# Second output product as three 256-column matmuls per group into one 256-column sum

## What is computed

```python
sig = 1.0 / (1.0 + np.exp(-f_logit))
f = lower_bound + (1.0 - lower_bound) * sig
h = f[:, t] * h + (1 - f[:, t]) * x[:, t]        # for every token t; y[:, t] = h
h1 = y @ w_in;   y1  = np.maximum(0.01 * h1, h1) @ w_out           # 256 -> 2048 -> 256
h2 = y1 @ w_in2                                                     # 256 -> 2048
g2 = np.where(h2 >= 1, h2, np.where(h2 <= -1, 0, (h2 + 1) ** 2 / 4))
out = g2 @ w_out2                                                   # 2048 -> 256
```

## Time and profile before

| | |
|---|---|
| median of 3 runs | 1105.47 us (1104.82 to 1106.61) |
| profiled execution, first to last instruction (span) | 1101.2 us |
| TensorE matmuls busy | 1078.7 us, 98%, 6156 matmuls, as many weight loads |
| VectorE busy | 813.1 us, 74% |
| ScalarE busy | 577.0 us, 52% |
| L686, 512 columns | 768 matmuls, 392 ns mean record |
| L691, 256 columns | 768 matmuls, 280 ns mean record |

### The profile page before, as it was taken

The page is one execution under the profiler, slowest core; times in us unless marked ns, Lnnn a source line. Parts: engine busy times, 40 slices in busy tenths (PEclk is TensorE's granted clock), DMA queues, the critical chain, the costliest instruction groups (busy, mean ns, idle before and its releaser), DMA issues.

```text
span 1101.2 us, 18595 instructions
## 1 busy us (share of the span) xinstructions
PE 1078.7 (98%) x6156; PEld 1041.4 (95%) x6156; DVE 813.1 (74%) x1542; ACT 577.0 (52%) x1210; POOL 42.7 (4%) x40
## 2 busy tenths in 40 slices
PE   4899999999999999999999999999999999999998
PEld 3899999999999999999999999999999999999997
DVE  5877777777777777777777777777777777777675
ACT  4545555555555555555555555555555555555453
POOL 5540000000000000000000000000000000000000
PEclk9999999999999999999999999999999999999999
DMA  5611020010100101010010200102001010000000
GB/s 166 172 54 30 1 44 1 14 29 14 29 0 16 27 14 29 0 29 14 14 29 0 43 0 14 29 0 43 0 14 29 14 24 0 14 0 15 1 15 13
DMA packets 105878, 27.36 MB, mean 25 GB/s; under 512 B 94272, under 2 KB 104704, under 8 KB 105856
## 3 DMA queue, kind: packets, MB, share of 16 engines
q1 hardware_dynamic: 104416, 22.36, 9.6%
q0 software_dynamic: 1440, 4.72, 1.3%
HBM read 20.84 MB, written 6.23 MB: 25 GB/s over the span
## 4 chain that ended last, share of the span: by engine, by line
PE 94%; DVE 3%; DMA 1%; SPq 1%; ACT 1%; issue 1%; DVEq 0%; ACTq 0%
PE H L657 47%; PE S L670 23%; PE S L686 16%; PE S L691 8%; SPq L254 1%; DMA bound<-in_lower_bound_dram 1%; DVE W L463 1%; DVE xT L495 0%; DMA raw<-in_moe_w_out_dram 0%; ACT W L331 0%; DVE X L510 0%; DVE H L536 0%; ACT G L389 0%; DVE G L542 0%; DVE late L528 0%
## 5 line engine op out<-in xcount | busy, mean ns | idle before, releaser
L657 PE MATMUL H<-X,W 128*128 (+2 forms) x1536 | 313.1, 339 | 13.9 <-DVE G L542 5.8
L657 PE MATMUL H<-Y,W 128*128 (+2 forms) x1536 | 309.3, 336 | 0.1
L670 PE MATMUL S<-G,W 128*128 128x384 f32 (+1 forms) x1536 | 308.3, 336 | 0.7 <-DVE Y L519 0.7
L382 ACT ACTIVATE leak<-H 128x384 f32<-128x384 f32 (+1 forms) x256 | 125.0, 488 | 321.8 <-PE H L657 311.5
L657 PEld LDWEIGHTS H<-X,W 128*128 128x128 f32 x1536 | 259.5, 189 | 27.2 <-issue 6.1
L686 PE MATMUL S<-W,G 128*128 128x512 f32 x768 | 278.1, 392 | 0.0
L670 PEld LDWEIGHTS S<-G,W 128*128 128x128 f32 x1536 | 270.8, 188 | 1.1 <-DVE G L542 1.0
L657 PEld LDWEIGHTS H<-Y,W 128*128 128x128 f32 x1536 | 270.2, 188 | 1.3 <-DVE G L564 0.8
L550 DVE SCALAR_TENSOR_TENSOR quad<-quad 128x384 f32<-128x384 f32 (+1 forms) x248 | 139.9, 564 | 118.3 <-ACT quad L396 118.2
L536 DVE TENSOR_TENSOR H<-H,leak 128x384 f32<-128x384 f32 (+1 forms) x256 | 143.6, 561 | 111.9 <-ACT leak L382 110.2
L691 PE MATMUL S<-W,G 128*128 128x256 f32 x768 | 214.9, 280 | 0.0
(11 more groups left out here) (38 smaller groups left out, 235.1 us busy)
## 6 DMA issues: line engine op xcount, KB each, us to landing
out_dram<-late SPq DMA_DIRECT2D x15, 384.0 KB, 2.4
stage_f<-in_f_logit_dram SPq DMA_DIRECT2D x56, 96.0 KB, 2.8
stage_x<-in_x_dram SPq DMA_DIRECT2D x56, 96.0 KB, 2.9
late<-in_moe_w_in_dram POOLq DMA_DIRECT2D x8, 256.0 KB, 3.2
late<-in_moe_w_out_dram POOLq DMA_DIRECT2D x8, 256.0 KB, 4.4
raw<-in_moe_w_in_dram SPq DMA_DIRECT2D x7, 256.0 KB, 4.2
raw<-in_moe_w_out_dram SPq DMA_DIRECT2D x7, 256.0 KB, 4.2
stage_f<-in_f_logit_dram SPq DMA_DIRECT2D x1, 384.0 KB, 3.4
```

The lines of the kernel that those rows point to most:

```text
L382: nc.scalar.activation(leak[:, 0:n], h1_bank(i, c)[:, 0:n], ACT.Copy, scale=0.01).then_inc(s_leak, 1)
L657: last = nc.tensor.matmul(bank[:, 0:n], w_in(W, a, c, k), V[:, parity(tile), b, k, 0:n], start=(k == 0 and (a, b) == PARTS[0]), stop=(k == ...
L670: last = nc.tensor.matmul(S1[:, d, 0:n], w_out(W1, a, c)[:, d * P:(d + 1) * P], G1[:, c % RING, b, 0:n], start=(c == 0 and (a, b) == PARTS ...
```

## The change

The two matmuls per group become the three of `PARTS`, each of 256 columns, all into `S2[:, g, 0:256]`: high G2 x high weights, high G2 x low weights, low G2 x high weights. The high part of G2 is now loaded twice per group. The columns 256 to 511 of the banks are no longer used, ScalarE's `cross_terms` with its buffer and semaphore is gone, and VectorE copies the sum to `result` in place of adding, waiting for TensorE's semaphores itself.

```diff
-        cross, result = late[:, 0], late[:, 1]
+        result = late[:, 1]
...
-            def cross_terms(tile):
-
-                reached(act, s_result, GROUPS * tile)
-                for g in range(GROUPS):
-
-                    if g < GROUPS - 1:
-                        act.wait_ge(s_sum2, (GROUPS - 1) * tile + g + 1)
-                    else:
-                        act.wait_ge(s_g2_used, CHUNKS * tile + CHUNKS)
-                    nc.scalar.activation(cross[:, g, :], S2[:, g, DIM:2 * DIM], ACT.Copy).then_inc(s_cross, 1)
-
...
-                    if s == O_STEP and not (static and not 0 <= i - 2 < TILES):
-                        cross_terms(i - 2)
...
-                    dve.wait_ge(s_cross, GROUPS * tile + g + 1)
-                    nc.vector.tensor_tensor(result[:, g, :], S2[:, g, 0:DIM], cross[:, g, :], ALU.add
-                                            ).then_inc(s_result, 1)
+                    if g < GROUPS - 1:
+                        dve.wait_ge(s_sum2, (GROUPS - 1) * tile + g + 1)
+                    else:
+                        dve.wait_ge(s_g2_used, CHUNKS * tile + CHUNKS)
+                    nc.vector.tensor_copy(result[:, g, :], S2[:, g, 0:DIM]).then_inc(s_result, 1)
...
-                    def high(start, stop):
-                        return nc.tensor.matmul(S2[:, g, :].rearrange("p (a d) -> p a d", a=2),
-                                                G2[:, c % RING, HI, tokens],
-                                                w_out(W2, slice(0, 2), c), start=start, stop=stop)
-
-                    def low():
-                        return nc.tensor.matmul(S2[:, g, 0:DIM], G2[:, c % RING, LO, tokens],
-                                                w_out(W2, HI, c), start=False, stop=False)
-
-
-                    if c < CHUNKS - 1:
-                        high(c == 0, False)
-                        last = low()
-                    else:
-                        low()
-                        last = high(False, True)
-                        if g < GROUPS - 1:
-                            last.then_inc(s_sum2, 1)
+                    for a, b in PARTS:
+                        last = nc.tensor.matmul(S2[:, g, 0:DIM], G2[:, c % RING, a, tokens], w_out(W2, b, c),
+                                                start=(c == 0 and (a, b) == PARTS[0]),
+                                                stop=(c == CHUNKS - 1 and (a, b) == PARTS[-1]))
+                    if c == CHUNKS - 1 and g < GROUPS - 1:
+                        last.then_inc(s_sum2, 1)
```

More of the change, by code:

```diff
@@ L198, in build @@
         s_sum2 = sem("s_sum2")
-        s_cross = sem("s_cross")
         s_result = sem("s_result")
```

## The result

The changed kernel takes 1109.55 us (median of nine runs, 1107.96 to 1113.59), the kernel before 1105.47 us (median of nine, 1102.21 to 1107.48). The ratio of the means is 1.0047, with a 95% interval of 1.0031 to 1.0064: slower by some 0.5%, or 3.4 to 7.1 us. The profiled executions have spans of 1106.9 and 1101.2 us, 5.7 us apart. Medians differ by 4.1 us, means by 5.2.

A forecast was written before the change was run, and what follows sets the result against it. The prediction took TensorE's distances between matmul starts as the bound. Its terms, +4.3 for instructions, -0.5 for the end and -0.2 in the last tile, gave 1105.47 + 3.6 = 1109.1 us, range 1105.2 to 1113.5.

The forecast's parts named there:

- The bound: Steady part: TensorE, busy 98% without waits, sets the time by distances between matmul starts; relieving ScalarE or VectorE buys nothing.
- Columns: Second product: each group keeps 768 columns, so nothing is gained or lost at 0.436 ns per column.
- Instructions: Second product: 768 more matmuls and loads, 5.6 ns per added matmul, +4.3 us.
- the prediction's own sign: Profile after, second product: nine matmuls take 1.055 us where 1.04 stood; other listed times would show the forecast wrong.
- rival C: Second product: adding into the same columns, or each load, costs: 120 ns each, 1115.6 us; chance 0.10 including values towards forecast.
- The upper bound: Most the added matmuls could cost: 120 ns each, read in a tile's last chunk, 10.8 us.
- rival B: Second product: keeping bank and shape makes matmuls cheaper, mean under 114.6 ns, 1103.1 us or less; chance 0.07.
- The end: End of the chain: the hop over ScalarE's copy goes, saving 0.5 us, at most 0.7.
- The 0.2 us in the last tile: TensorE's 0.40 us stall in the last tile: faster VectorE copies give back 0 to 0.4 us, 0.2 taken.
- A: Second product: the part per matmul is small, distance near 116 ns, costing 1.5 us; 1106.3 us, no measurable change; chance 0.18.
- D: Second product: loads or instruction supply can't hold 117 ns over nine; at 130 ns +33.8 us, 1138.6 us; chance 0.05.
- The 4.3 us between the median and the profiled span: Kernel before: median 1105.47 us lies 4.3 us above the profiled span, taken as launch and end, unchanged.

The follow-up runs named there:

- the end alone: Kernel before with its matmuls kept, ScalarE's copy gone and VectorE copying only columns 0 to 255, so one product is left out: ratio 0.9995, tile 67.34 us.
- the split alone: Kernel before with only the 512-column matmul split into two of 256; ScalarE still copies, VectorE still adds: ratio 1.0045, span 1109.7 us, tile 67.74 us.

## Why the prediction was right, point by point

**The bound.** Right. TensorE stayed the bound with no waits in the steady part, the clock didn't move, and relieving ScalarE was worth nothing there (67.34 us per tile with the end alone).

**Columns.** Right as a statement: the loss comes with the split, wherever the halves go.

**Instructions.** That three matmuls of 256 columns cost more than the pair was right, the size too small: 8.3 ns for each added matmul with its load, not 5.6, so 6.4 us, not 4.3. This is the term that was off. By the prediction's own sign, nine matmuls take 1.07 us, between the 1.055 of the forecast and the 1.08 of rival C. The forecast priced three matmuls of 256 columns at the 117.2 ns that one costs after a 512-column one. In a row they cost 118.9, so a group takes 356.7 ns in place of 346.0 to 347.0, about 10 ns; the step after gets a little of it back, and 8.3 remain: on average nine take 1.0701 us and the six before 1.0414, and the `up` behind them 1.0525 in place of 1.0552. Why 256 columns take 118.9 ns here was not found. In the run with three of 512 and then three of 256 the latter took 116 ns on average, so a row of equal sizes is not the reason by itself. A fixed part per instruction of 5.6 ns is not shown either: equal matmuls differ by up to 9 ns with their place (173 to 182 ns at 384 columns, 115 to 122 at 256; the same nine took 1.0742 us in the run with 240 and 144), and the 5.6 ns is what a line through two means of such distances gave.

The upper bound was read from the right place: the last chunk's 120 ns was nearer to 118.9 than the mean of 688 was. The trace's starts at that place give 115, 120 and 120 ns for the three 256-column matmuls, so the reading of 110 ns, which spoke for rival B, was rounding. That the turned order of that chunk is the reason is argued, not shown.

The page TensorE: Matmul & The Clock Gate of the Trainium skill, section "Back-to-back issue gap", has 2.5 ns for each matmul beside its columns; the measured 8.3 ns is over three times that, so the formula doesn't fit this kernel, where each matmul brings a load. The section itself calls it the gap of an isolated matmul and says that in a stream of loads and matmuls both set the spacing, which the prediction left out. The 107 ns for a load, from that page's section "LDWEIGHTS (loading the stationary operand)" (128/1.2), comes near the pace of 111 to 112 ns that matmuls of 128 and 192 columns kept.

**The end.** 0.5 us for the hop over ScalarE was right. The 0.2 us in the last tile wasn't there: the forecast took VectorE's copy to be perhaps faster than its add, and it is as long (417 against 416 ns on average). In the last tile the three copies take 1.08 us, as long as the adds (1.07). TensorE's longest wait there went from 0.4 to 0.3 us all the same, but it did so with the adds kept (0.3 in the split alone), so that 0.1 us isn't the copies' doing.

**The rivals.** A (a small part per matmul) and B (faster when bank and shape stay) fell with the tile's 0.40 us; the runs with another bank and another order of loads (67.74 and 67.73 us) show that neither bank nor repeated load enters. C had two causes. Adding into the same columns fell with them; a price of the load under each matmul was not tested apart, and C's direction, more than 117 ns in a row, was right. D (the loads can't hold the pace) fell for 256 columns, but by 7 ns only: at 128 or 192 columns the loads do set the pace, and the kernels take 1347.7 and 1182.3 us.

**The number, and luck.** The forecast of 1109.1 us is 0.45 under the measured median, closer than its working deserves. The instruction term was 2.1 us too small and the 0.2 us of the last tile were not there. With the terms as measured (6.4 - 0.5, and the start earlier by 0.1) the same sum gives 1105.5 + 5.8 = 1111.3 us. Medians differ by only 4.1 us and means by 5.2; the start of the kernel, which scatters by up to 6 us from run to run, is enough for such differences, and they can't be told further. The 4.3 us between the median and the profiled span were not launch and end either: every run of the changed kernel takes some 1.8 us more than its own span, so the profiled execution of the kernel before was a short one.

## What to carry to other kernels

Where TensorE is the bound and each matmul brings its own weight load, count matmuls as well as columns: here each one more cost 8.3 ns when 512 columns became two of 256, but 48 to 49 ns when 384 became two of 192 or 240 and 144 (224 and 225 in place of 176), and 104 when 256 became two of 128 (223 in place of 119), since a matmul with its load took 111 to 113 ns on average in all of these. A split was cheap only where both pieces were long enough to cover a load; between 192 and 256 no size was measured alone. Price a matmul from rows where its neighbours are those it will have; a mean over a different mixture was 1.7 ns too low, and it entered three times per group. Judge a change of a few nanoseconds by the length of the whole tile: it can show up in a neighbouring piece that was not touched, as in the run with the 512-column matmuls first. Work that is covered on VectorE or ScalarE is worth only what it adds to the very end, and a longer instruction in the same place can use the cover up.

## What was not expected of the hardware

A matmul of 128 columns and one of 192, fp32r operands with a 128x128 load each, both take 111 to 112 ns, and a pair of 240 and 144 takes 225 ns, as much as two loads' pace and one nanosecond. In all three the loads start about 112 ns apart within the cut piece, whatever the matmuls do.

Equal matmuls don't have one price. Those of 384 columns go through a turn of five distances, 173, 174, 175, 182 and 176 ns (176.0 on average), and an edit elsewhere in the step decides how often the 182 falls into a piece of six. Adding into the same columns, the same bank or another bank, and loading the same block twice running, make no difference at 256 columns (67.73 to 67.74 us per tile).
